# Attention scores over each head's own 64 partitions, one bank per head, queries packed, one score buffer instead of two

## The chip, the core and the metric

The kernel runs on one core of one Trainium2 chip. The metric is the device time of one execution in microseconds (us); lower is better.

## What is computed

Three layers follow one another: windowed attention with block summaries, a mixture of experts with one expert per token, and a Fourier mixing layer with a normalised two-layer network. The change touches only the first. Cut to that part, the reference is:

```python
B, H, S, D = 2, 8, 768, 64          # block 32, window 16
k_sum = k.reshape(B, H, nb, block, D).max(axis=3)
v_sum = v.reshape(B, H, nb, block, D).mean(axis=3)
scores_l = scale * q @ k.T          # kept where |i - j| < 16
scores_s = scale * q @ k_sum.T + log(block)
a = softmax(concat([masked scores_l, scores_s]))
out = a @ concat([v, v_sum])
# then: expert layer on out, then the Fourier layer
```

## The kernel before

The kernel is written engine by engine, with semaphores set and waited for by hand; on each engine, instructions run in the order of the code. The engines are TensorE (PE, whose weight loads stand apart as PEld), VectorE (DVE), ScalarE (ACT), GpSimd (POOL) and SyncE (SP), which issues most transfers.

Attention goes over 8 pairs of heads (`PAIRS`), the two heads of a pair side by side on 128 partitions: head 0 on partitions 0 to 63, head 1 on 64 to 127. Each pair has 6 tiles of 128 queries (`ST`), so there are 48 tiles. The first four pairs run in a loop of two pairs per turn; the last four are written out, and between their tiles stand the gate's logits of the expert layer and the routing that follows from them (`after_probs`, `after_masks`, `after_outputs` on DVE, `beside` on PE).

One tile passes through these steps:

- `scores` (PE, L1697): for each head one matmul of 128 queries against 184 keys (160 in the window, 24 block maxima). The query tile `qT[:, par, hh, ...]` has all 128 partitions, with zeros on the 64 of the other head, so that a contraction over 128 partitions gives one head's scores. An f32 matmul is two passes in the trace, so a tile's scores are four rows of L1697. Both heads of tile t lie side by side in the PSUM bank `S_BANK[t % 2]`.
- `mask_scores` (DVE, L943): adds the mask of each head and takes the row minimum into `masked`; a short read of the accumulator follows each. It signals `masked_ok`.
- exponentials (ACT, L706): two per tile, from `masked` to `probs`, each with a read of its sum.
- `turn_probs` (PE, L1706): three transposes of the probabilities, which DVE copies out (L952, `probs_out`).
- `values` (PE, L1720 to L1722): the product with the values, which DVE normalises (L973).

On PE the step of tile t in a pair is: `turn_probs(t)`, `scores(t + 2)`, for t below 3 a third of the next pair's query and key transposes (`stage`, L1670), work of the gate in the written-out pairs, then `values(t - 1)`. On DVE it is: copy of tile t's transposed probabilities, `mask_scores` of tile t + 2, normalisation of tile t - 1, and after tile 2 the block maxima of the next pair (L932).

`stage` on ACT copies the transposes out of PSUM, scaling the queries: one copy of the first 512 keys (L679), then 256 keys (L683) and 256 queries (L686), then 512 queries (L686). The two L686 copies are each made twice, 64 partitions at a time, since each head has its own zero-padded `qT`. DVE clears `qT` once, at the start (L920).

Of the kernel before, what the change touches and what calls it, by code (L numbers as in the profile page):

```python
# [11 lines left out]
ACT = mybir.ActivationFunctionType  # L12
# [3 lines left out]
B, H, S, D = 2, 8, 768, 64  # L16
BLOCK, WINDOW = 32, 16
DM = H * D
E, FE = 8, 1024
FM = 4 * DM  # L20
P = 128
NB = S // BLOCK
ST = S // P
NT = B * ST
TOK = B * S
PAIRS = B * H // 2
HP = H // 2
SCALE = float(D) ** -0.5


PRE = WINDOW - 1
WK = 160
WB = WK - P
NS = WK + NB
# [12 lines left out]
XW = 516  # L47
# [111 lines left out]
def build(nc, q, k, v, w1, w2, ch1, ch2, consts, four, out):  # L159
    cols = shape_constants()[0]  # L160
    ctx = ExitStack()
    with ctx:
# [28 lines left out]
        mask = const("mask").rearrange("p (v h s) -> p v h s", v=3, h=2)  # L191
# [12 lines left out]
        a = Cut(arena)  # L204
        q_raw = a(ST * P).rearrange("p (t h d) -> p t h d", t=ST, h=2)
        k_raw = a(ST * P).rearrange("p (t h d) -> p t h d", t=ST, h=2)

        qT = a(4 * S).rearrange("p (b h n) -> p b h n", b=2, h=2)
        kT = a(KTW)

        k_win = a(2 * ST * KW).rearrange("p (b t n) -> p b t n", b=2, t=ST)
# [28 lines left out]
        r = Cut(parts)  # L240
# [423 lines left out]
        def _(act):  # L664
# [10 lines left out]
            def stage(i, par, piece):  # L675

                act.wait_ge(qk_ps, 3 * i + piece + 1)
                if piece == 0:
                    act.activation(kT[:, PRE:PRE + 512], Q_BANK[:, :], ACT.Copy).then_inc(qk_sb, 1)  # L679
                    return  # L680
                lo, n, at = (0, 256, 256) if piece == 1 else (256, 512, 0)
                if piece == 1:
                    act.activation(kT[:, PRE + 512:PRE + S], Q_BANK[:, 0:256], ACT.Copy)  # L683
                for hh in range(2):
                    r = slice(D * hh, D * hh + D)
                    last = act.activation(qT[r, par, hh, lo:lo + n], Q_BANK[r, at:at + n], ACT.Copy, scale=-SCALE)  # L686
                last.then_inc(qk_sb, 1)

            def block_mean_rows(i, par):

# [207 lines left out]
        def _(dve):  # L898
# [17 lines left out]


            dve.memset(unspent[:, 0:1], 1.0)
            for tile in (qT, probs, xa[:, :, DM + 2:XW], kT[:, 0:PRE], oh, capped[:, 0:1]):
                dve.memset(tile, 0.0)  # L920
            dve.memset(table_i[:, :], 0)
            link(dve.memset(kT[:, PRE + S:KTW], 0.0))
# [11 lines left out]
            def mask_scores(i, par, t):  # L934

                u = ST * i + t
                slot = 12 * par + 2 * t
                var_ = 0 if t == 0 else 2 if t == ST - 1 else 1
                dve.wait_ge(s_ps, u + 1)
                dve.wait_ge(probs_ok, u + 1)  # L940
                dve.sem_inc(waited, 1)
                for hh in range(2):
                    last = dve.tensor_tensor_reduce(out=masked[:, t % 3, hh, :], in0=S_BANK[t % 2][:, NS * hh:NS * hh + NS], in1=mask[:, var_, hh, :],  # L943
                                                    scale=1.0, scalar=3.0e38, op0=ALU.add, op1=ALU.min, accum_out=neg_max[:, slot + hh:slot + hh + 1])
                last.then_inc(masked_ok, 1)

# [715 lines left out]
        def _(pe):  # L1662
# [25 lines left out]
            def scores(i, par, t):  # L1688
                if t == 0:
                    pe.wait_ge(qk_sb, 3 * i + 3)  # L1690
                    pe.wait_ge(kwin_ok, i + 1)
                    pe.wait_ge(ksum_ok, i + 2)

                pe.wait_ge(masked_ok, ST * i + t + 1)

                for hh, keys in ((0, slice(KS, KW)), (1, slice(0, NS))):
                    last = pe.matmul(S_BANK[t % 2][:, NS * hh:NS * hh + NS], qT[:, par, hh, P * t:P * t + P], k_win[:, par, t, keys],  # L1697
                                     start=True, stop=True)
                last.then_inc(s_ps, 1)

# [85 lines left out]
            def attend(i, par, last_pair):  # L1786
                for t in range(ST):
# [9 lines left out]
                    if t:  # L1797
                        values(i, par, t - 1)
                    if isinstance(i, int) and (i, t) in BEHIND:
                        logits(BEHIND[i, t])  # L1800
                    if isinstance(i, int) and (i, t) in GATE_TURN:
                        turn_gate(GATE_TURN[i, t])
# [259 lines left out]
```

## Time and profile before

| | |
|---|---|
| median of 3 runs | 635.12 us (634.58 to 637.52) |
| time of the profiled execution | 639.09 us |
| its span (first to last instruction) | 637.0 us |
| mean granted TensorE clock | 0.991 |
| PE busy | 604.4 us, 95% |
| PEld busy | 497.5 us, 78% |
| DVE busy | 339.9 us, 53% |
| ACT busy | 248.6 us, 39% |
| POOL busy | 127.1 us, 20% |
| PE's share of the chain that ended last | 78% |

Busy time is the sum of an engine's instructions, overlaps counted once. The span is some 2 us shorter than the time because launch and end lie around it. PE's busy share is an average over three very different layers; what the change is worth has to be read in the attention stage, which ends near 128 us. The chain that ended last goes back from the last instruction, at each step to what released it.

### The profile page before, as it was taken

What the parts mean: (1) busy time and instruction counts of PE and PEld (TensorE: products, weight loads), DVE (VectorE), ACT (ScalarE), POOL (GpSimd) and SP (SyncE); (2) the same over time, 40 slices, a digit from 0 to 9 for tenths busy, and PEclk for the clock granted to TensorE, in tenths of its full rate; (3) what the DMA queues carried; (4) which work ended last, traced back from release to release, by engine and by line L of the source; (5) the groups of instructions that cost most, each with busy time, mean ns of one, the idle gap of its engine ahead of it and who ended that gap; (6) DMA issues with size and microseconds to landing.
All of it is one profiled execution on the core that took longest, in us unless ns stands there. A gap on an engine that the chain in (4) does not pass through costs nothing.

```text
span 637.0 us, 10225 instructions
## 1 busy us (share of the span) xinstructions
PE 604.4 (95%) x3072; PEld 497.5 (78%) x3073; DVE 339.9 (53%) x902; ACT 248.6 (39%) x542; POOL 127.1 (20%) x154
## 2 busy tenths in 40 slices
PE   4899999899989999999799999999999999999997
PEld 3799998788767888888644678888888888888886
DVE  4888679678563564532180665454533344533333
ACT  3588776465132462311011533334333333333331
POOL 5665545403701000000100411200500000200000
PEclk9999999799989999999999999999999999999999
DMA  6967742686536543611232250000010000100001
GB/s 158 167 143 158 157 90 65 242 267 255 204 130 241 179 141 132 241 33 33 99 131 98 101 199 1 1 1 1 26 41 1 2 0 1 66 1 0 2 1 66
DMA packets 59304, 61.68 MB, mean 97 GB/s; under 512 B 42688, under 2 KB 42816, under 8 KB 58240
## 3 DMA queue, kind: packets, MB, share of 16 engines
q1 hardware_dynamic: 54384, 47.21, 25.2%
q0 software_dynamic: 3440, 11.32, 4.7%
q10 hardware_dynamic: 1440, 2.64, 1.4%
q8 instruction: 21, 0.34, 0.3%
q14 instruction: 19, 0.16, 0.1%
HBM read 48.27 MB, written 12.89 MB: 96 GB/s over the span
## 4 chain that ended last, share of the span: by engine, by line
PE 78%; DVE 6%; issue 5%; DMA 4%; ACT 2%; SPq 2%; another core or an unknown queue 1%; POOL 1%; DVEq 0%; ACTq 0%; POOLq 0%
PE bank L2003 21%; PE bank L2016 20%; PE bank L1859 10%; PE bank L1834 9%; PE bank L1697 2%; PE bank L1918 2%; PE bank L1706 1%; ACT arena L706 1%; PE bank L1921 1%; PE bank L1967 1%; DVE parts L1387 1%; PE bank L1846 1%; DMA sorted_x<-zero_row,small 1%; PE bank L1976 1%
## 5 line engine op out<-in xcount | busy, mean ns | idle before, releaser
L2003 PE MATMUL bank<-parts 128*128 128x512 f32 x576 | 139.4, 391 | 1.6 <-DVE parts L1387 1.6
L2016 PE MATMUL bank<-parts 128*128 128x512 f32 x576 | 138.2, 389 | 0.0
L2003 PEld LDWEIGHTS bank<-parts 128*128 128x128 f32 x576 | 107.4, 188 | 24.0 <-DVE parts L1387 1.8
L2016 PEld LDWEIGHTS bank<-parts 128*128 128x128 f32 x576 | 108.1, 188 | 22.5
L1387 DVE TENSOR_TENSOR parts<-arena,parts 128x512 fp32r<-128x512 f32 (+1 forms) x108 | 77.0, 744 | 79.5 <-ACT parts L863 75.8
L1834 PE MATMUL bank<-parts 128*128 128x512 f32 x312 | 77.2, 400 | 2.7 <-issue 1.8
L1859 PE MATMUL bank<-parts 128*128 128x512 f32 x312 | 74.5, 394 | 4.1 <-DVE parts L1387 3.8
L1834 PEld LDWEIGHTS bank<-parts 128*128 128x128 f32 x312 | 58.2, 191 | 16.3 <-issue 4.6
L1859 PEld LDWEIGHTS bank<-parts 128*128 128x128 f32 x312 | 57.6, 188 | 16.6 <-issue 2.5
L863 ACT ACTIVATE parts<-arena 128x512 fp32r<-128x512 f32 x48 | 30.3, 631 | 82.9 <-PE bank L2016 82.9
L1645 DVE SCALAR_TENSOR_TENSOR parts<-bank,parts 128x512 fp32r<-128x512 f32 x48 | 33.2, 691 | 48.2 <-ACT parts L888 48.2
L888 ACT ACTIVATE parts<-bank 128x512 fp32r<-128x512 f32 x48 | 28.7, 598 | 69.3 <-PE bank L2003 67.8
L1387 DVE TENSOR_TENSOR parts<-bank,parts 128x512 fp32r<-128x512 f32 x52 | 34.4, 686 | 27.7 <-ACT parts L853 20.7
L706 ACT ACTIVATE arena<-arena,small 128x184 f32<-128x184 f32 x96 | 42.1, 440 | 16.1 <-DVE small L943 15.3
L1697 PE MATMUL bank<-arena 128*128 128x184 f32 x192 | 41.8, 345 | 1.8 <-ACT arena L686 1.3
L602 POOL DMA_INDIRECT folded_y<-mid,dest_i x13 | 12.6, 973 | 126.7 <-DVE dest_i L1498 126.4
L558 POOL TENSOR_TENSOR mid<-mid 128x1024 f32<-128x1024 f32 (+3 forms) x28 | 33.7, 1204 | 11.9 <-DVE small L1371 8.2
L1697 PEld LDWEIGHTS bank<-arena 128*128 128x128 f32 x192 | 32.6, 207 | 3.0 <-ACT arena L686 1.7
L798 ACT ACTIVATE parts<-bank 128x512 fp32r<-128x512 f32 x26 | 14.1, 594 | 52.5 <-PE bank L1846 40.4
L943 DVE CUSTOM_DVE_ANT_0 arena<-bank,cst 128x184 f32<-128x184 f32 x96 | 29.3, 342 | 9.3 <-PE bank L1697 7.2
L1497 DVE TENSOR_SCALAR mid<-bank,small 128x512 f32<-128x512 f32 x13 | 9.7, 750 | 40.6 <-PE bank L1859 34.5
L858 ACT ACTIVATE parts<-arena 128x512 fp32r<-128x512 f32 x48 | 29.7, 618 | 0.0
(218 smaller groups left out, 764.9 us busy)
## 6 DMA issues: line engine op xcount, KB each, us to landing
mid<-in_moe_w SPq DMA_DIRECT2D x16, 512.0 KB, 6.6
arena<-in_moe_w SPq DMA_DIRECT2D x16, 512.0 KB, 6.5
arena<-in_moe_w_ch SPq DMA_DIRECT2D x2, 2048.0 KB
arena<-in_moe_w_ch SPq DMA_DIRECT2D x4, 1024.0 KB, 9.5
arena<-in_k SPq DMA_DIRECT2D x16, 192.0 KB, 3.2
arena<-in_q SPq DMA_DIRECT2D x16, 192.0 KB, 3.9
mid<-in_v SPq DMA_DIRECT2D x16, 192.0 KB
x_all<-folded_y SPq DMA_DIRECT2D x6, 512.0 KB, 6.4
```

Of the source, the lines that this page charges most:

```text
L558: pool.tensor_tensor(blocks[:, par, 0:n], blocks[:, par, 0:n], blocks[:, par, n:2 * n], ALU.add).then_inc(halved, 1)
L706: last = act.activation(probs[:, t % 3, (2 * NSP - NS) * hh:(2 * NSP - NS) * hh + NS], masked[:, t % 3, hh, :], ACT.Exp, scale=-1.0, bias= ...
L858: act.activation(m1_hi[:, f % 2, :].rearrange("p (c n) -> p c n", c=DC), m1_raw[:, :, P * f:P * f + P], ACT.Copy).then_inc(m1h_ok, 1)
L863: act.activation(m2_hi[:, f % 2, :], m2_raw[:, f, :], ACT.Copy).then_inc(m2h_ok, 1)
L943: last = dve.tensor_tensor_reduce(out=masked[:, t % 3, hh, :], in0=S_BANK[t % 2][:, NS * hh:NS * hh + NS], in1=mask[:, var_, hh, :], scale ...
L1387: return dve.tensor_tensor(out, whole, upper.bitcast(F32), ALU.subtract)
L1645: dve.scalar_tensor_tensor(g_lo[:, f % 2, :], bank[2 + f % 2][:, 0:GN], 0.0, g_hi[:, f % 2, :].bitcast(F32), ALU.max, ALU.subtract).then_i ...
L1697: last = pe.matmul(S_BANK[t % 2][:, NS * hh:NS * hh + NS], qT[:, par, hh, P * t:P * t + P], k_win[:, par, t, keys], start=True, stop=True)
L1834: last = pe.matmul(bank[1 + half][:, :], x[:, r], w[:, c, f], start=(c == 0 and x is xT_hi and w is w1_hi), stop=(c == DC - 1 and w is w1_lo))
L1859: last = pe.matmul(bank[5][:, :], x[:, c, :], w[:, c // 2, f], start=(c == 0 and x is hT_hi and w is w2_hi), stop=(c == FC - 1 and w is w2 ...
L2003: last = pe.matmul(bank[2 + f % 2][:, 0:GN], w[:, f % 2, r], x[:, par, c, :], start=(c == 0 and w is m1_hi and x is cT_hi), stop=(c == DC ...
L2016: last = pe.matmul(bank[4 + t][:, :], x[:, f % 2, r], w[:, f % 2, :], start=(f == 0 and x is g_hi and w is m2_hi), stop=(f == MC - 1 and w ...
```

## The change

Three things change together. The queries of both heads are kept in one packed tile `qT[:, par, n]`, head 0 on the lower 64 partitions and head 1 on the upper 64, and ACT copies both with one instruction; nothing needs zeros any more, so the clearing of `qT` goes. Each score matmul contracts over the 64 partitions of its own head. And each head writes to a bank of its own, `S_BANK[0]` or `S_BANK[1]`, for every tile: two banks still, but one buffer for a tile's scores instead of two. So `scores` of a tile waits until the tile before it is masked, where it waited for the one before that; and the logits that use a score bank in the last pair wait for the last mask.

```diff
-        qT = a(4 * S).rearrange("p (b h n) -> p b h n", b=2, h=2)
+        qT = a(2 * S).rearrange("p (b n) -> p b n", b=2)
...
-                for hh in range(2):
-                    r = slice(D * hh, D * hh + D)
-                    last = act.activation(qT[r, par, hh, lo:lo + n], Q_BANK[r, at:at + n], ACT.Copy, scale=-SCALE)
-                last.then_inc(qk_sb, 1)
+                act.activation(qT[:, par, lo:lo + n], Q_BANK[:, at:at + n], ACT.Copy, scale=-SCALE).then_inc(qk_sb, 1)
...
-            for tile in (qT, probs, xa[:, :, DM + 2:XW], kT[:, 0:PRE], oh, capped[:, 0:1]):
+            for tile in (probs, xa[:, :, DM + 2:XW], kT[:, 0:PRE], oh, capped[:, 0:1]):
...
-                    last = dve.tensor_tensor_reduce(out=masked[:, t % 3, hh, :], in0=S_BANK[t % 2][:, NS * hh:NS * hh + NS], in1=mask[:, var_, hh, :],
+                    last = dve.tensor_tensor_reduce(out=masked[:, t % 3, hh, :], in0=S_BANK[hh][:, 0:NS], in1=mask[:, var_, hh, :],
...
-                pe.wait_ge(masked_ok, ST * i + t + 1)
+                pe.wait_ge(masked_ok, ST * i + t + THREE)
 
                 for hh, keys in ((0, slice(KS, KW)), (1, slice(0, NS))):
-                    last = pe.matmul(S_BANK[t % 2][:, NS * hh:NS * hh + NS], qT[:, par, hh, P * t:P * t + P], k_win[:, par, t, keys],
+                    r = slice(D * hh, D * hh + D)
+                    last = pe.matmul(S_BANK[hh][:, 0:NS], qT[r, par, P * t:P * t + P], k_win[r, par, t, keys],
                                      start=True, stop=True)
                 last.then_inc(s_ps, 1)
...
                     if isinstance(i, int) and (i, t) in BEHIND:
+                        pe.wait_ge(masked_ok, ST * PAIRS + THREE)
                         logits(BEHIND[i, t])
```

Hardly an instruction moves. On TensorE the order in the loop stays; here is the step of tile 3 before (transposes of the probabilities L1706, scores L1697, values L1720 to L1722; bank numbers are those of PSUM):

```order
L1706 MATMUL bank4<-cst,arena 128x128 [waits pT_sb,probs_ok]
L1706 MATMUL bank4<-cst,arena 128x128 x2
L1697 MATMUL bank1<-arena 128x184 [waits masked_ok]
L1697 MATMUL bank1<-arena 128x184
L1720 MATMUL bank5<-arena 128x128 [waits att_out,pT_sb]
L1721 MATMUL bank5<-arena 128x64
L1722 MATMUL bank5<-arena 128x64
```

The same step of the changed kernel, whose lines are renumbered (L1704, L1695, L1718 to L1720):

```order
L1704 MATMUL bank4<-cst,arena 128x128 [waits pT_sb,probs_ok]
L1704 MATMUL bank4<-cst,arena 128x128 x2
L1691 REGISTER_ALU
L1695 MATMUL bank0<-arena 128x184 [waits masked_ok]
L1695 MATMUL bank1<-arena 128x184
L1718 MATMUL bank5<-arena 128x128 [waits att_out,pT_sb]
L1719 MATMUL bank5<-arena 128x64
L1720 MATMUL bank5<-arena 128x64
```

The two score matmuls now go to two banks, and the value that `masked_ok` is waited for is higher by two, which is one tile later: that wait now stands for the mask of the tile just before.

On ScalarE the query copies of a pair (L686 before) stand between the exponentials (L706), before:

```order
L683 ACTIVATE arena<-bank 128x256 [waits qk_ps]
L686 ACTIVATE arena<-bank 64x256 x2
L703 REGISTER_ALU
L706 ACTIVATE arena,small<-arena,small 128x184 [waits pT_ps,masked_ok]
L706 ACTIVATE arena,small<-arena,small 128x184
L677 REGISTER_ALU
L686 ACTIVATE arena<-bank 64x512 [waits qk_ps]
L686 ACTIVATE arena<-bank 64x512
```

and in the changed kernel (L684 and L703):

```order
L683 ACTIVATE arena<-bank 128x256 [waits qk_ps]
L684 ACTIVATE arena<-bank 128x256
L700 REGISTER_ALU
L703 ACTIVATE arena,small<-arena,small 128x184 [waits pT_ps,masked_ok]
L703 ACTIVATE arena,small<-arena,small 128x184
L677 REGISTER_ALU
L684 ACTIVATE arena<-bank 128x512 [waits qk_ps]
```

Two copies of a pair are gone; nothing else moves there.

## Rows read from the trace of the kernel before

**Rows 1.** Busy time by engine in three stretches (calls), granted clock, DMA share, GB/s.
```profile
45.00:70.00 25.00, 24.69 (x200) 24.06 (x199) 20.95 (x96) 20.52 (x69) 16.10 (x26) 1.00 0.73 157
70.00:95.00 25.00, 24.93 (x212) 24.27 (x212) 17.09 (x81) 17.84 (x59) 10.34 (x18) 1.00 0.48 104
95.00:120.00 25.00, 21.42 (x162) 19.89 (x160) 20.84 (x120) 14.49 (x51) 13.97 (x19) 0.95 0.32 99
```

**Rows 2.** The same view, score matmuls alone: PE and PEld busy (passes).
```profile
0.00:20.00 20.00, 4.26 (x12) 3.50 (x12) 1.00 0.79 162
20.00:93.00 73.00, 27.07 (x132) 20.78 (x132) 1.00 0.65 137
93.00:127.00 34.00, 10.46 (x48) 8.28 (x48) 0.90 0.50 157
```

**Rows 3.** Timeline of PE over one pair: start, duration, line, shape, passes.
```profile
44.92 0.79 PE L1697 MATMUL bank<-arena 128*128 128x184 f32 x4
45.54 0.60 PE L1670 MATMUL bank<-cst,arena 128*128 128x128 f32 x4
45.98 0.49 PE L1706 MATMUL bank<-cst,arena 128*128 128x128 f32 x3
46.31 0.79 PE L1697 MATMUL bank<-arena 128*128 128x184 f32 x4
...
50.34 0.79 PE L1697 MATMUL bank<-arena 128*128 128x184 f32 x4
...
51.36 0.39 PE L1722 MATMUL bank<-arena 128*128 128x64 f32 x2
51.91 0.55 PE L1706 MATMUL bank<-cst,arena 128*128 128x128 f32 x3 [0.17 <-ACT arena L706]
52.34 0.89 PE L1697 MATMUL bank<-arena 128*128 128x184 f32 x4
...
56.30 0.79 PE L1697 MATMUL bank<-arena 128*128 128x184 f32 x4
```

**Rows 4.** Timeline of PE in the Fourier layer, rows used*columns of the array ahead of the shape.
```profile
352.55 1.03 PE L1967 MATMUL bank<-arena 128*128 128x258 f32 x4
353.52 0.70 PE L1968 MATMUL bank<-cst,arena 1*128 1x258 f32 x2
354.15 1.14 PE L1976 MATMUL bank<-arena 128*128 128x258 f32 x4
355.12 1.03 PE L1967 MATMUL bank<-arena 128*128 128x258 f32 x4
```

**Rows 5.** Timeline of the weight loads (PEld) at the same place.
```profile
353.52 0.29 PEld L1968 LDWEIGHTS bank<-cst,arena 1*128 1x128 f32 x2 [0.34 <-issue]
354.14 0.73 PEld L1976 LDWEIGHTS bank<-arena 128*128 128x128 f32 x4 [0.34 <-issue]
```

**Rows 6.** Timeline of PE behind six 8-row transposes.
```profile
97.76 0.49 PE L1720 MATMUL bank<-arena 128*128 128x128 f32 x2
98.08 0.33 PE L1721 MATMUL bank<-arena 128*128 128x64 f32 x2
```

**Rows 7.** Groups by line and shape up to 190 us: ACT's copies of `stage`.
```profile
L686 ACT ACTIVATE arena<-bank 64x512 f32<-64x512 f32 x16 | 9.5, 592 | 2.0 <-PE bank L1670 1.8
L686 ACT ACTIVATE arena<-bank 64x256 f32<-64x256 f32 x16 | 6.0, 372 | 0.1
L679 ACT ACTIVATE arena<-bank 128x512 f32<-128x512 f32 x8 | 4.8, 598 | 10.4 <-PE bank L1670 10.4
```

**Rows 8.** Timeline of DVE, last reads of the masks of tiles 2 and 5.
```profile
46.55 0.08 DVE L943 DVE_READ_ACCUMULATOR2_ANT small<- 128x1 f32 x1
...
52.53 0.08 DVE L943 DVE_READ_ACCUMULATOR2_ANT small<- 128x1 f32 x1
```

**Rows 9.** Timeline of the start.
```profile
1.46 2.62 DVE L920 MEMSET arena<- 128x3072 f32 x1 [0.61 <-issue]
...
6.28 0.60 ACT L679 ACTIVATE arena<-bank 128x512 f32<-128x512 f32 x1 [0.39 <-PE bank L1670]
...
20.36 0.90 PE L1670 MATMUL bank<-cst,arena 128*128 128x128 f32 x3 [2.88 <-DMA arena<-in_k]
```

**Rows 10.** The chain that ended last, in order of time, behind the attention.
```profile
121.55 7.45 DMA sorted_x<-zero_row,small
...
134.17 5.79 DMA arena<-in_moe_w
```

## The prediction

> **What bounds the kernel now.** I read the busy time by stretch first, because the average over three layers says nothing of one stage. From 45 to 95 us PE is busy 24.7 and 24.9 of every 25 us, while DVE has 17 to 21 and ACT 18 to 21 [rows 1]: the first two thirds of the attention are PE's alone. From 95 to 120 us PE falls to 21.4 and DVE has 20.8: there the two take turns, because routing work stands between the masks. Counting score passes by the same stretches, four to a tile, 3 tiles are computed before 20 us, 33 from 20 to 93, and 12 after [rows 2]. The wait that ends the start is a transfer: PE stands at 20.36 us for the second pair's keys [rows 9], so whatever happens before that is worth nothing. Behind the attention the chain goes through the clearing of rows (7.45 us) and the first expert weights (5.79 us) [rows 10]; both are triggered by the routing that is threaded through the last pairs, and the weights also wait for the last scores, since they overwrite the attention's buffers. So I carry a shift of the attention to the end one for one.
>
> Then the timeline of one pair in the loop, from scores at 44.92 to the same place at 56.30: 11.38 us [rows 3]. Starts, not durations, give the pace. Scores 44.92 to 45.54: 0.62 us for four passes of 184 columns, 0.155 each, with no gap, so the weight loads are hidden. `stage` takes 0.44, the transposes 0.33. Once per pair PE waits: the values' last two passes start at 51.36 and pace out at about 51.58, the next transposes start at 51.91, 0.33 us late, released by an exponential; they and the scores behind them take 0.43 and (from the duration, 0.89 for 0.79) 0.72 instead of 0.33 and 0.62. That is some 0.5 us of waiting and restarting per pair.
>
> **The change part by part.**
>
> *Scores over 64 rows.* No row of this kernel uses 64 rows. The nearest are matmuls over 1 row between matmuls over 128 [rows 4]. Undisturbed, 258 columns pace at 0.217 us a pass: (1.03 − 0.38)/3, where 0.38 is the last pass's duration. From 352.55 to 355.12 there are ten passes, 2.17 us, but 2.57 us go by. The 0.40 us of excess splits into about 0.10 behind L1967 (0.97 for four), 0.20 in L1968 (0.63 for two) and 0.10 in L1976 (0.97 for four). The loads show why: the first load of L1968 and of L1976 starts together with the matmul, 0.34 us after the load before it [rows 5], where elsewhere it is done ahead. The array empties (about 0.1), then loads uncovered (about 0.1), once going in and once coming out. The 8-row transposes show the second half too: L1720 behind them takes 0.32 instead of the usual 0.22 [rows 6]. Each tile's scores now stand between 128-row work on both sides, so each pays this: +0.40 us.
>
> The Trainium skill, "TensorEngine Tiling (Array Packing)", Key Properties, says the same: changing the tiling mode, not just the tile, drains TensorE. By that rule 64 rows would pay as 1 row does; by a reading in which only a very short contraction pays, the term would be nothing. The rows decide only for 1 and 8 rows.
>
> Against that stands overlap. The two heads now use different halves of the array. The passes come in the order head 0, head 0, head 1, head 1. If a pass can run beside one of the other half but starts in order, only the second and third overlap: at most one pass, 0.155 us. None is the other bound. The loads (0.11 us each, by the pace of the transposes) must also come one after another: head 1's first load, the third in the row, ends at 0.33 us, while the second pass runs from about 0.26 to 0.42. Some 0.1 is left to overlap; I take 0.10. Net per tile: +0.30, between +0.245 and +0.40.
>
> *Waits inside a pair.* The 0.5 us that PE waits now for the exponential is absorbed: PE comes later by more than that, and ACT comes earlier, since the second 64-partition query copies go. A copy costs the same over 64 as over 128 partitions (592 and 598 ns), so ACT saves 0.59 + 0.37 = 0.96 us per pair [rows 7]. Beyond the absorbed wait this is worth nothing, ACT having 4 us of idle in 25.
>
> Now the single buffer. `scores(3)` must wait for the mask of tile 2, which ends at 46.63 against scores at 46.31; the first scores of the next pair wait for the mask of tile 5, which ends at 52.61 against 52.34 [rows 3, 8]. With 0.05 for the signal these are 0.37 and 0.32 us late in today's schedule. Elsewhere in a pair `values` and longer steps stand between, and the mask is done. What is queued behind the waiting scores is everything of PE: the transposes, the values, and through them DVE's normalisation. In the new schedule PE reaches `scores(3)` up to 0.3 us later than now while the mask moves less, so that wait shrinks; at the next pair's first scores PE is held up by 0.3 more per tile but no longer by the exponential, so that wait stays. I take 0.5 per pair for both, between 0 and 0.75. It cancels the absorbed 0.5.
>
> So +0.30 × 6 = +1.8 us per pair, 0.30 per tile. For 33 tiles: +9.9. For the 12 tiles behind 93 us PE has room, but a slower score also delays the mask that DVE waits for; I take half, 0.15: +1.8, between 0 and 0.40 each.
>
> *The rest.* The clearing of 3072 columns, 2.62 us of DVE, is gone; the first key copy of ACT waits for PE's transposes until 6.28 anyway, and PE stands for the transfer at 20.36 [rows 9]: nothing. Were that transfer 2 us earlier, it would still be nothing. The added waits before two logits in the last pair stand where the last masks are long done. The DVE masks keep size and number.
>
> Sum: 9.9 + 1.8 = 11.7 us. On the profiled execution, 639.09 becomes 650.8. That execution is 4.0 us above the median of 635.12; on the median the same sum gives **646.8**, forecast 647.
>
> **The rivals.**
>
> *Slower, as above (0.75).* Its own range: low, one full pass of overlap (+0.245), no new waits while 0.5 a pair is absorbed (−0.08 a tile), nothing in the last 12: 33 × 0.16 = 5.3, so 640.4. High, no overlap (+0.40), waits of 0.75 a pair less 0.5 absorbed (+0.04), and the last 12 in full: 33 × 0.44 + 12 × 0.40 = 19.3, so 654.4.
>
> *Faster: the heads run side by side (0.12).* If 64-row tiles neither drain nor expose loads, and both passes of one head run beside those of the other, scores take 0.31 instead of 0.62. For it: the layout, halves of the array and separate banks, is what such overlap needs. Against it: the order of passes and [rows 4]. PE would gain 0.31 a tile, but would then meet the mask sooner: about 0.17 a tile goes into the single buffer's waits. 45 × 0.14 = 6.3, so 629. It decides when entering and leaving costs less than about 0.15 us a tile together. The Trainium skill, "TensorE: Matmul & The Clock Gate", Part 3, speaks for it: matmuls of different row groups are said to start about 4 ns apart. No row here shows it.
>
> *No change (0.13).* The switch is free or nearly so, and one pass overlaps: −0.155 a tile, given back by the new waits (0.75 a pair, 0.125 a tile). 45 × −0.03 = −1.4, so 634. The same result comes if both heads overlap fully and the switch costs 0.15. For it: the switch is seen only at 1 and 8 rows.
>
> **How the numbers follow.** About 0.5%, 3.2 us, is what a measurement of this kernel can tell from none. The range must leave out no more than 2 in 10: it leaves out the faster rival and a little above the high bound, and takes in no change from 637 and up: 637 to 655. Almost all of the likeliest case is over 638.3: slower 0.75, same 0.13, faster 0.12.
>
> **What would show it.** In the changed profile: scores marked 64*128; from the first score pass to the next group's start 0.7 to 0.8 us instead of 0.62; the first load of scores and that of the group behind starting with their matmuls, with idle before them; 12.8 to 13.6 us a pair instead of 11.38; PE waiting for the mask before `scores(3)` and the next pair's first; ACT's L684 at 16 calls instead of 32, no time won by it. Wrong would be: score starts of the two heads a few ns apart, or loads still hidden at the change of rows (then the faster rival); or a pair near 11.4 us with new waits for the mask (no change); or a delay of the attention that the weight transfers swallow.

## The result, and the profile after

| | before | after |
|---|---|---|
| median of 20 runs | 635.75 us (632.72 to 640.04) | 638.37 us (636.14 to 640.72) |
| ratio, with its 95% interval | | 1.0041 (1.0026 to 1.0056) |
| time and span of the profiled execution | 639.09 and 637.0 us | 638.82 and 636.8 us |
| PE, DVE, ACT busy | 604.4, 339.9, 248.6 us | 603.1, 338.2, 240.5 us |

The change costs 2.6 us, 0.4%: slower, but within the 0.5% that I had called no change. I had forecast 11.7 us more. Medians and ratios in this document leave out the executions that ran in a slower state of the chip, three of the ten of `maxima_earlier_copies_as_before` and one of the kernel before beside them.

The busy time by stretch, in the changed kernel; the columns are those of [rows 1].

```profile
45.00:70.00 25.00, 23.81 (x193) 18.97 (x192) 20.07 (x91) 17.88 (x66) 15.51 (x24) 1.00 0.73 155
70.00:95.00 25.00, 25.00 (x211) 21.34 (x209) 16.37 (x79) 15.62 (x52) 10.10 (x18) 1.00 0.39 87
95.00:120.00 25.00, 22.27 (x181) 17.63 (x181) 23.26 (x126) 14.37 (x52) 14.97 (x21) 1.00 0.41 116
```

In the loop's stretch PE is busy for 23.8 of 25 us where it was 24.7: PE now waits, and not for a transfer. Timeline of PE around the pair of [rows 3]. The rows begin one tile earlier than those did: 44.08 is the place that is 42.67 in the kernel before (scores of this pair's tile 1), and the next scores, at 46.41, are those that stood at 44.92.

```profile
44.08 0.58 PE L1695 MATMUL bank<-arena 64*128 64x184 f32 x4
...
47.41 0.49 PE L1704 MATMUL bank<-cst,arena 128*128 128x128 f32 x3
48.08 0.58 PE L1695 MATMUL bank<-arena 64*128 64x184 f32 x4 [0.18 <-DVE small L940]
48.59 0.66 PE L1667 MATMUL bank<-cst,arena 128*128 128x128 f32 x4
49.09 0.39 PE L1718 MATMUL bank<-arena 128*128 128x128 f32 x2
...
51.75 0.50 PE L1704 MATMUL bank<-cst,arena 128*128 128x128 f32 x3
52.18 0.58 PE L1695 MATMUL bank<-arena 64*128 64x184 f32 x4
52.69 0.49 PE L1718 MATMUL bank<-arena 128*128 128x128 f32 x2
53.02 0.33 PE L1719 MATMUL bank<-arena 128*128 128x64 f32 x2
...
53.41 0.50 PE L1704 MATMUL bank<-cst,arena 128*128 128x128 f32 x3
54.42 0.58 PE L1695 MATMUL bank<-arena 64*128 64x184 f32 x4 [0.51 <-DVE small L940]
...
56.08 0.58 PE L1695 MATMUL bank<-arena 64*128 64x184 f32 x4
```

The shape 64*128 says that half of the array's rows are used. Three readings of starts:

- Scores last 0.51 us to the next group (52.18 to 52.69), where they lasted 0.62. They got shorter.
- The transposes ahead of them last 0.43 (51.75 to 52.18), where 0.33 was usual: +0.10. The values behind them take 0.33 for their first two passes (52.69 to 53.02), where 0.22 was usual: +0.10. With `stage` behind them it is 0.50 (48.59 to 49.09) for 0.44: some +0.05.
- Scores come late twice, for the mask (L940). The scores of tile 3: 47.41 + 0.43 is 47.84, and they start at 48.08, 0.24 late. The first scores of the next pair: 53.41 + 0.43 is 53.84, and they start at 54.42, 0.58 late. No wait for an exponential is left.

The weight loads at the same place show the rest of it:

```profile
51.64 0.37 PEld L1704 LDWEIGHTS bank<-cst,arena 128*128 128x128 f32 x3
52.18 0.30 PEld L1695 LDWEIGHTS bank<-arena 64*128 64x128 f32 x4 [0.17 <-issue]
52.69 0.30 PEld L1718 LDWEIGHTS bank<-arena 128*128 128x128 f32 x2 [0.21 <-issue]
```

The loads of scores and of the group behind both start together with their matmuls, as at the one-row matmuls of [rows 5]: the array empties first, and then the first load is uncovered, going in and coming out.

The rows above merge the four passes of a tile's scores. Taken one by one, the trace has their starts at 52.181, 52.187, 52.441 and 52.447 us, and those of their loads at 52.179, 52.186, 52.287 and 52.294. The passes come in twos, 6 ns apart, and so do the loads. The trace doesn't say which head a pass is of; I take one of each two for each head. A start of the two heads a few ns apart is what the prediction had named as the sign that it was wrong.

The pair from 44.08 to 56.08 takes 12.00 us for 11.38. The other pairs of the loop that show in full take 11.82 and 11.83; the wait at the scores of tile 3 is only 0.07 there, the other one as long as here. In the written-out pairs, taken from scores of tile 2 to scores of tile 2, the steps are 18.22, 14.26 and 14.16 for 18.05, 13.76 and 14.14.

A wait stands at the start too, in the first pair, just behind the transfer of the second pair's keys. The kernel before:

```profile
20.36 1.12 PE L1670 MATMUL bank<-cst,arena 128*128 128x128 f32 x4 [2.88 <-DMA arena<-in_k]
21.91 1.44 PE L1697 MATMUL bank<-arena 128*128 128x184 f32 x4
```

and the changed kernel:

```profile
19.87 1.11 PE L1667 MATMUL bank<-cst,arena 128*128 128x128 f32 x4 [3.80 <-DMA arena<-in_k]
22.56 0.98 PE L1695 MATMUL bank<-arena 64*128 64x184 f32 x4 [0.93 <-DVE small L940]
```

From the first transposes behind the transfer to the scores of tile 3 it is 2.69 us for 1.55. DVE is as late in both kernels, since it computes block means until then, but with two buffers PE did not have to wait for it. So 1.1 us of the loss arise before the loop is under way.

Where all that leads, in rows of the timelines, first of the kernel before:

```profile
91.98 0.79 PE L1697 MATMUL bank<-arena 128*128 128x184 f32 x4
107.10 0.94 DVE L932 TENSOR_REDUCE arena<-arena 128x24 f32<-128x768 f32 x1
...
116.23 0.29 DVE L973 TENSOR_TENSOR x_all<-bank,small 128x128 f32<-128x128 f32 x1 [2.58 <-remote]
```

and of the changed kernel:

```profile
95.00 0.58 PE L1695 MATMUL bank<-arena 64*128 64x184 f32 x4
110.24 0.94 DVE L929 TENSOR_REDUCE arena<-arena 128x24 f32<-128x768 f32 x1
```

The same scores come 3.0 us later, and the last block maxima 3.1 us later. Read at a tile's scores, the shift is 1.05 us early in the second pair (33.54 and 34.59), 2.6 three pairs on (67.67 and 70.24) and 3.3 at 113.62 and 116.88. The medians differ by 2.6 us, so most of that shift reaches the end; as medians and profile are of different executions, no row shows it being carried. The two profiled spans, 637.0 and 636.8, don't show the loss, because the execution profiled of the kernel before lost 2.58 us at 116.23 to a wait whose cause the trace only calls remote. PE stood still behind it for 2.05 us, and its granted clock from 117 to 124 us was 0.53, for 1.00 in the changed kernel. The other profile has no such wait. So the medians are compared for the sum, and not these two spans.

### The profile page after: what moved, and what is told of

It reads as the page before. It is cut to its first block, busy times and chain, and to the rows that moved or that the text cites. A ratio compares the mean times of both kernels' runs of the same rounds, so it can differ in the third digit from the quotient of the medians.

```text
span 636.8 us, 10206 instructions
## 1 busy us (share of the span) xinstructions
PE 603.1 (95%) x3072; PEld 478.9 (75%) x3073; DVE 338.2 (53%) x901; ACT 240.5 (38%) x526; POOL 127.4 (20%) x154
## 4 chain that ended last, share of the span: by engine, by line
PE 84%; DVE 5%; DMA 4%; issue 4%; ACT 1%; POOL 1%; DVEq 0%; SPq 0%; ACTq 0%; POOLq 0%
PE bank L2002 21%; PE bank L2015 20%; PE bank L1858 11%; PE bank L1833 10%; PE bank L1695 2%; PE bank L1917 2%; PE bank L1667 2%; DMA x_all<-sorted_x 2%; PE bank L1920 1%; PE bank L1718 1%; PE bank L1845 1%; PE bank L1966 1%; DMA sorted_x<-zero_row,small 1%; PE bank L1736 1%; PE bank L1704 1%
## 5 line engine op out<-in xcount | busy, mean ns | idle before, releaser
L703 ACT ACTIVATE arena<-arena,small 128x184 f32<-128x184 f32 x96 | 42.0, 440 | 19.2 <-DVE small L940 18.6
L1695 PE MATMUL bank<-arena 64*128 64x184 f32 x192 | 29.6, 386 | 7.1 <-DVE small L940 6.2
L940 DVE CUSTOM_DVE_ANT_0 arena<-bank,cst 128x184 f32<-128x184 f32 x96 | 29.5, 344 | 7.3 <-PE bank L1695 3.9
L949 DVE COPY arena<-bank 128x384 f32<-128x384 f32 x48 | 26.5, 552 | 3.2 <-PE bank L1704 2.5
```

The lines of the kernel that those rows point to most:

```text
L703: last = act.activation(probs[:, t % 3, (2 * NSP - NS) * hh:(2 * NSP - NS) * hh + NS], masked[:, t % 3, hh, :], ACT.Exp, scale=-1.0, bias= ...
L1695: last = pe.matmul(S_BANK[hh][:, 0:NS], qT[r, par, P * t:P * t + P], k_win[r, par, t, keys], start=True, stop=True)
```

## The experiments

Each median stands beside runs of the kernel before on the same chip, and the ratio is to those. The pair times are from scores of tile 1 to scores of tile 1 of the next pair (44.08 to 56.08 above), the three of the loop that show in full; before, they are 11.38 us each.

| kernel | median us | ratio to before | us a pair |
|---|---|---|---|
| after | 638.37 | 1.0041 (1.0026 to 1.0056) | 11.82, 12.00, 11.83 |
| single_buffer_only | 642.43 | 1.0104 (1.0084 to 1.0125) | 12.31, 12.38, 12.30 |
| each_head_twice | 652.05 | 1.0232 (1.0199 to 1.0266) | 13.78, 13.80, 13.77 |
| copies_and_clearing_as_before | 640.38 | 1.0060 (1.0040 to 1.0080) | 11.83, 12.00, 11.82 |
| four_banks_in_loop | 639.34 | 1.0056 (1.0038 to 1.0074) | 11.69, 11.94, 11.70 |
| scores_behind_values | 648.03 | 1.0190 (1.0168 to 1.0213) | 12.21 each |
| block_maxima_earlier | 635.75 | 0.9986 (0.9967 to 1.0005) | 11.25, 11.42, 11.25 |
| maxima_and_mask_earlier | 635.36 | 0.9977 (0.9957 to 0.9996) | 11.24, 11.25, 11.25 |
| before_with_dve_moves | 638.78 | 1.0030 (1.0014 to 1.0046) | 11.99 each |
| before_with_maxima_earlier | 643.79 | 1.0030 (0.9992 to 1.0068) | 12.06, 11.99, 11.99 |
| maxima_earlier_copies_as_before | 645.36 | 1.0074 (1.0044 to 1.0104) | 12.05, 12.23, 12.04 |

For the last two the kernel before beside them took 642.26 and 640.70 us, so that only their ratios and pair times compare with the others.

### How the heads overlap

**single_buffer_only** is the kernel before with one buffer and a bank for each head, still over 128 rows: the part that was to cost waits, alone.

```diff
-                pe.wait_ge(masked_ok, ST * i + t + 1)
+                pe.wait_ge(masked_ok, ST * i + t + THREE)
-                    last = pe.matmul(S_BANK[t % 2][:, NS * hh:NS * hh + NS], qT[:, par, hh, P * t:P * t + P], k_win[:, par, t, keys],
+                    last = pe.matmul(S_BANK[hh][:, 0:NS], qT[:, par, hh, P * t:P * t + P], k_win[:, par, t, keys],
```

> The kernel before with one part of the change: each head has a score bank of its own for every tile and so one buffer, but scores still contract over 128 partitions with zero-padded queries, and ACT's split copies stay. Theory: in the changed kernel the waits for the mask are what costs, about 0.7 us a pair, since PE stands at the scores of tile 3 and at the next pair's first. Then this one is slower than before by 3 to 6 us (639 to 642), and its scores take 0.62 us a tile as before, with two waits for a mask per pair of 0.3 us each. Rival: the wait is absorbed by the wait for the exponential, and the switch of rows is the whole cost: 635 to 637.

It measured 12.3 us a pair and a ratio of 1.0104: slower than the whole change. Scores were late for the mask twice a pair, and the transposes at 56.06, 0.31 us behind the pace, still stand for the exponential (the gap is too short for a bracket):

```profile
50.38 0.89 PE L1697 MATMUL bank<-arena 128*128 128x184 f32 x4 [0.22 <-DVE small L943]
...
55.53 0.39 PE L1722 MATMUL bank<-arena 128*128 128x64 f32 x2
56.06 0.55 PE L1706 MATMUL bank<-cst,arena 128*128 128x128 f32 x3
56.84 0.89 PE L1697 MATMUL bank<-arena 128*128 128x184 f32 x4 [0.23 <-DVE small L943]
```

So one buffer costs 0.9 to 1.0 us a pair by itself, and the rest of the change wins 0.4 to 0.5 of it back, although by the rows above it gives PE 0.3 to 0.4 us a pair more to do: what shrinks is the waiting. (The query copies have no part in that: copies_and_clearing_as_before, below.) In my forecast the halved rows were the loss and the buffer nothing on balance; the larger loss is the buffer's. No run has the halved rows with the two score buffers of the kernel before and all else as it was.

**each_head_twice** computes each head's scores twice over, in the order head 0, head 0, head 1, head 1 (eight passes; the second result replaces the first).

```diff
-                    last = pe.matmul(S_BANK[hh][:, 0:NS], qT[r, par, P * t:P * t + P], k_win[r, par, t, keys],
-                                     start=True, stop=True)
+                    for _ in range(2):
+                        last = pe.matmul(S_BANK[hh][:, 0:NS], qT[r, par, P * t:P * t + P], k_win[r, par, t, keys],
+                                         start=True, stop=True)
```

> The changed kernel with each head's score matmul issued twice in a row into the same bank (the second repeats the first), so the order is head 0, head 0, head 1, head 1 by instruction, eight passes a tile. It asks how the passes of the two halves of the array overlap. Theory: each half works through its own passes regardless of the order in the code, so eight passes take four pass times, 0.62 us, and the scores take 0.51 + 0.31 = 0.82 us from their start to the next group's; whole kernel about 12 us over the changed one, 648 to 652. Rival: only passes that are neighbours overlap (head 0's second with head 1's first), so that of four instructions the outer two run alone: 0.31 + 0.31 + 0.31 + 0.2 = 1.13 us a tile; 660 and over.

Timeline of PE:

```profile
56.31 0.90 PE L1696 MATMUL bank<-arena 64*128 64x184 f32 x8
57.14 0.66 PE L1667 MATMUL bank<-cst,arena 128*128 128x128 f32 x4
```

Eight passes take 0.83 us from start to start, four took 0.51: four more passes for 0.32, two passes' time. Had the four passes of head 1 started only behind the last of head 0, at most one would have been hidden: 7 × 0.155 + 0.2 is 1.29; my rival's 1.13 is excluded too. One by one the passes again start in twos, 13 ns apart: 56.310 and 56.323, 56.570 and 56.583, 56.726 and 56.739, 56.882 and 56.895. The halves each work through their own passes, whatever stands between them in the code.

**both_heads_lower_half** takes head 1's operands from the lower 64 partitions too. It computes scores from head 0's data twice and none of head 1's; so the attention's output differs, the routing with it, and only its attention stage can be read. It was measured twice.

```diff
-                    r = slice(D * hh, D * hh + D)
+                    r = slice(0, D)
```

> The changed kernel with the second head's score matmul reading partitions 0 to 63 as well (so the second head's scores are computed from the first head's data). Same number of passes, same 64-row shape, same banks and waits, but both heads use the same half of the array and can't run side by side. Theory: the changed kernel's 0.51 us a tile holds two pass times (0.31) and 0.2 of drain and load; without overlap four pass times: 0.82 us. 45 tiles by 0.31 is 14 us, less what the waits for the mask take back: 647 to 653. Rival (the prediction's bound, at most one pass overlaps): 0.66 us a tile, 643 to 646. Rival (64 rows are simply cheap, no overlap in it): 638, no change.

> The kernel with both heads' scores on partitions 0 to 63 once more (second head's scores computed from the first head's data), for a trace with TensorE at its full pace in the attention. Only the attention is read, since the routing depends on the data. Theory: 0.82 us from the start of a tile's scores to the next group's, 0.31 more than in the changed kernel, and about 13 us a pair. Rival (at most one pass had overlapped): 0.66 us.

The first time its six executions took 649.5 to 703.08 us, so that the forecast of 647 to 653 says nothing, and in the profiled one PE was at half pace through the loop, until about 100 us: 24.1 us a pair. The second time (one execution, 659.17 us) that lasted until about 56 us, timelines of PE and of the weight loads:

```profile
47.60 1.59 PE L1695 MATMUL bank<-arena 64*128 64x184 f32 x4
49.12 1.11 PE L1667 MATMUL bank<-cst,arena 128*128 128x128 f32 x4
...
56.36 0.90 PE L1695 MATMUL bank<-arena 64*128 64x184 f32 x4
57.19 0.49 PE L1718 MATMUL bank<-arena 128*128 128x128 f32 x2
...
56.36 0.61 PEld L1695 LDWEIGHTS bank<-arena 64*128 64x128 f32 x4 [0.33 <-issue]
```

From 56.36 on the pace is the usual one, and there four passes on one half last 0.83 us, against 0.51 on two halves. That is 0.32 or two passes, with the same switch, the same number of loads and the same banks: the overlap is that of the halves, and it is whole. The four loads span 0.61 us on one half and 0.30 on two, so they run side by side as well. The pair takes 13.7 us there where I expected about 13; up to 1.1 us of it is the lengthened DVE operation described under before_with_maxima_earlier.

### Where the new wait comes from

**four_banks_in_loop** gives the pairs of the loop two score buffers again (four banks), taking a bank from the transposed probabilities, which keep one.

```diff
+        def score_bank(i, t, hh):
+            return (bank[2], bank[4])[hh] if looped(i, t) and t % 2 else S_BANK[hh]
...
-                pe.wait_ge(masked_ok, ST * i + t + THREE)
+                pe.wait_ge(masked_ok, ST * i + t + (1 if looped(i, t) else THREE))
```

> The changed kernel with two buffers of scores for the four pairs of the loop: odd tiles use PSUM banks 2 and 4, and the transposed probabilities use bank 3 alone there. The last four pairs are as in the changed kernel. Theory: the waits for the mask at scores go in the loop, some 0.7 us a pair, in 3.5 pairs: 11.2 to 11.4 us a pair instead of 12.0, 635.5 to 637. Rival: the single buffer costs nothing, or DVE's masks are late anyway and the wait only moves to the transposes: 638, no change.

```profile
52.61 0.52 PE L1714 MATMUL bank<-cst,arena 128*128 128x128 f32 x3 [0.33 <-DVE arena L959]
53.06 0.58 PE L1705 MATMUL bank<-arena 64*128 64x184 f32 x4
```

No wait for a mask is left in the loop. The transposes wait for DVE's copy of the ones before (L959) in its place, and the pair is shorter by 0.1 us only. DVE was late, and whichever bank it has to free next shows it. By itself this run can't tell whether banks are scarce, since one of the two that the scores got was taken from the transposes; block_maxima_earlier, below, shows that one buffer will do once DVE is earlier.

**scores_behind_values** puts `scores(t + 2)` at the end of PE's step, behind `values(t - 1)`, so that the mask has longer.

```diff
-                    if t + 2 < ST:
-                        scores(i, par, t + 2)
...
+                    if t + 2 < ST:
+                        scores(i, par, t + 2)
```

> The changed kernel with PE's order in a tile's step changed: scores of tile t + 2 stand behind the values of tile t - 1 instead of ahead of them, still single-buffered. Theory: PE does 0.6 us of other work before it needs the mask, so the waits for the mask go, while the exponential of tile t + 2 still has more than a tile's time: 633 to 636. Rival: the mask, the exponential and with them the transposes come 0.6 us later, and the wait only moves from scores to transposes, or grows: 638 to 642.

```profile
53.85 0.58 PE L1695 MATMUL bank<-arena 64*128 64x184 f32 x4
54.74 0.55 PE L1704 MATMUL bank<-cst,arena 128*128 128x128 f32 x3 [0.31 <-ACT arena L703]
```

Later scores make a later mask and a later exponential, and the transposes wait instead, here and once more in each pair (0.21 us at 56.94). The pair takes 12.21 us and the ratio is 1.0190. The loop explains 1 to 2 of some 9.5 us by which this kernel is slower than the changed one; the rest lies behind the loop, where among others three waits of 0.45 us for ACT (L736) come up at 81.54, 85.16 and 88.79, and was not taken apart.

**block_maxima_earlier** changes only DVE: the block maxima of the next pair (0.95 us, once a pair) go ahead of the normalisation of tile 1 instead of behind it.

```diff
+                    if t == 2 and not last_pair:
+                        block_max(i + 1, 1 - par)
                     if t:
                         normalise(i, par, t - 1, out_at(t - 1))
                     if isinstance(i, int):
                         after_outputs(i, t)
-                    if t == 2 and not last_pair:
-                        block_max(i + 1, 1 - par)
```

> The changed kernel with one thing moved on DVE: the block maxima of the next pair stand ahead of the normalisation of tile 1 instead of behind it, where DVE idles 0.5 us for the values. Theory: they and all behind them come 0.5 us earlier, so the mask of tile 5 is done when PE reaches the next pair's first scores, and that wait (0.58 us a pair) goes: 11.4 to 11.5 us a pair instead of 12.0, 634 to 636. Rival: the wait moves on to the transposes of tile 5, which need the exponential: 637 to 638.5.

The reason is in DVE's timeline of the changed kernel:

```profile
52.06 0.29 DVE L970 TENSOR_TENSOR x_all<-bank,small 128x128 f32 x1 [0.49 <-PE bank L1720]
52.28 0.95 DVE L929 TENSOR_REDUCE arena<-arena 128x24 f32<-128x768 f32 x1
...
53.21 0.55 DVE L949 COPY arena<-bank 128x384 f32<-128x384 f32 x1
...
53.76 0.32 DVE L940 CUSTOM_DVE_ANT_0 arena<-bank,cst 128x184 f32<-128x184 f32 x1
```

DVE stands 0.49 us for the values, then does the maxima, and only then the copy and the mask for which PE's scores at 54.42 wait. With the maxima in the idle time (49.84 there, ahead of L970 at 50.71), the time is that of the kernel before (0.9986, 0.9967 to 1.0005), and PE's rows at the same places are

```profile
51.77 0.50 PE L1704 MATMUL bank<-cst,arena 128*128 128x128 f32 x3
52.20 0.58 PE L1695 MATMUL bank<-arena 64*128 64x184 f32 x4
52.72 0.49 PE L1718 MATMUL bank<-arena 128*128 128x128 f32 x2
```

with no wait for the next pair's first scores. The pair takes 11.25 us, or 11.42 where the scores of tile 3 wait (0.18 idle at 46.44). That is about what the terms give without a new wait: 11.38 − 0.5 (the old wait) + 0.4 (rows) = 11.28.

**maxima_and_mask_earlier** adds a second move on DVE in the loop: the mask of tile 2 ahead of the copy of tile 0.

> As the kernel before it in this call, and in the loop's pairs the mask of tile 2 stands ahead of the copy of tile 0's transposed probabilities instead of behind it. Theory: that mask starts when its scores are done, 0.2 us earlier, and PE's wait at the scores of tile 3 (0.1 to 0.24 us) goes as well: 0.1 to 0.2 us a pair less than the kernel with the maxima alone in four pairs, a difference too small to be told in the time (under 1 us) but seen in the pair's period. Rival: the copies come later and PE waits for them at the values or transposes: equal or longer period.

It makes all pairs 11.25 and the ratio 0.9977 (0.9957 to 0.9996). That is ahead of the kernel before by 0.2%, barely clear of its interval, and not to be told from the maxima alone.

### Whether the kernel before could have the same

**before_with_dve_moves** is the kernel before with both moves, and **before_with_maxima_earlier** with that of the maxima alone.

> The control: the kernel before, with the same two moves on DVE (block maxima ahead of the normalisation of tile 1, mask of tile 2 ahead of the copy of tile 0). Theory: the kernel before doesn't wait for masks, so the moves are worth nothing there (within 1 us of before, 11.3 to 11.4 us a pair), and what they won in the changed kernel was the price of the single buffer. Rival: the moves shorten DVE's work order as such and win 2 to 3 us here too, so that the changed layout is no better than before with them.

> The kernel before with one of the two moves on VectorE alone: the block maxima of the next pair ahead of the normalisation. It has two score buffers, so its masks are not waited for by TensorE, and its one wait of 0.5 us a pair is for an exponential. If the loss of the kernel before with both moves (11.99 us a pair) came from the mask of tile 2 going ahead of the copy of tile 0, then this kernel keeps 11.38 us a pair and 636 us, within 0.3%. If the block maxima are what harms it (the normalisation later by a microsecond, hence the values and the exponentials), the pair stays near 12.0 us and the time near 639. If they help it as they helped the changed kernel, the pair falls to 11.2 and the time to 634, and then the changed kernel with the same move has nothing that the kernel before could not have.

Both take 11.99 us a pair for 11.38: the move that helps the changed kernel lengthens the pair of the one before, and the maxima alone do it. The time of the first is 0.3% up; that of the second has the same ratio, but an interval that reaches 1. DVE's timeline of the second, and below it ACT's:

```profile
55.01 1.18 DVE L960 TENSOR_SCALAR small<-small 128x4 f32<-128x4 f32 x1
56.11 0.55 DVE L952 COPY arena<-bank 128x384 f32<-128x384 f32 x1
```

```profile
53.83 0.19 ACT L706 ACTIVATION_READ_ACCUMULATOR arena<-arena,small 128x1 f32 x1
...
55.12 0.45 ACT L706 ACTIVATE arena<-arena,small 128x184 f32<-128x184 f32 x1
...
55.91 0.19 ACT L706 ACTIVATION_READ_ACCUMULATOR arena<-arena,small 128x1 f32 x1
```

L960 is an operation of 0.16 us on the exponentials' sums of tiles 4 and 5. Here it holds DVE for 1.18, the copy behind it is late, and PE waits for that copy (0.48 us at 56.71). The expectations call this a wait for the sums, and the rows say otherwise: the read that ends tile 5's exponentials is over at 54.02, and DVE passed the semaphore that stands for it at 54.84, ahead of L960. What runs beside L960 is the exponential of the next pair's tile 0 (55.12 to 56.10), whose sums it doesn't read. In the loops of five kernels the operation took 1.14 to 1.27 us, 19 times, two kernels with packed copies among them (each_head_twice and both_heads_lower_half_again). Each time it had started between 0.18 us ahead of that exponential and 0.04 us behind its start, and it ended 0.1 to 0.3 us behind its last read. In the changed kernel it starts 0.30 us ahead (56.17 and 56.47) and takes 0.16. So the loss hangs on where two engines' operations meet in time. What holds the operation is not shown.

**copies_and_clearing_as_before** is the changed kernel with each query copy made twice, 64 partitions at a time, and with the clearing; **maxima_earlier_copies_as_before** has the earlier maxima too.

```diff
-                act.activation(qT[:, par, lo:lo + n], Q_BANK[:, at:at + n], ACT.Copy, scale=-SCALE).then_inc(qk_sb, 1)
+                for hh in range(2):
+                    r = slice(D * hh, D * hh + D)
+                    last = act.activation(qT[r, par, lo:lo + n], Q_BANK[r, at:at + n], ACT.Copy, scale=-SCALE)
+                last.then_inc(qk_sb, 1)
```

> The changed kernel with ACT's query copies split into two of 64 partitions again and with 3072 columns cleared at the start again; nothing of PE's or the banks is touched. Theory: neither was worth anything, since PE waits for DVE's masks and not for ACT, and the start ends with a transfer: 638 to 639.5, no change beyond 1 us. Rival: the packed copies shorten the path to the exponentials of tile 4 and with it pay for part of the rest: 641 to 643, and waits of PE for ACT of 0.3 us a pair come back.

> The changed kernel with the block maxima ahead of the normalisation (which alone gave 11.25 to 11.42 us a pair) and with the query copies made twice, 64 partitions at a time, and the queries cleared, as before. In the kernel before, the same move of the block maxima made a pair 11.99 us: there the query copies of 1.19 us stand between the exponentials, and the check of the exponentials' sums waited 1.1 us with the copy of the last transposes behind it. If the longer query copies are what turns the move into a loss, this kernel shows about 11.9 us a pair, that wait of VectorE again, and a time near 639. If the copies are hidden here too (they made no difference to the pair without the move: 11.83 and 12.00 against 11.82 and 12.00), the pair stays at 11.25 to 11.4 and the time near 636, and the loss of the kernel before with the move comes from its slower scores over 128 rows.

Without the move the doubled copies change no pair (11.83, 12.00, 11.82); the ratio is 0.2% (1.2 us) above that of the changed kernel, with intervals that overlap, so it stays open whether the clearing at the start is worth anything. With the move they cost 0.8 us a pair (12.05 for 11.25). ACT's timeline of that kernel, and below it DVE's:

```profile
52.57 1.20 ACT L687 ACTIVATE arena<-bank 64x512 f32<-64x512 f32 x2
...
57.10 0.45 ACT L707 ACTIVATE arena<-arena,small 128x184 f32<-128x184 f32 x1
...
57.89 0.19 ACT L707 ACTIVATION_READ_ACCUMULATOR arena<-arena,small 128x1 f32 x1
```

```profile
57.05 1.14 DVE L961 TENSOR_SCALAR small<-small 128x4 f32<-128x4 f32 x1
```

The long operation of 1.1 us on DVE is back, beside the next pair's first exponential as in the kernel before. So the packed copies are what lets the earlier maxima pay here: doubled, the copies cost a pair nothing while DVE is late, and 0.8 us once it is not. The 0.8 is not ACT's 0.96 us handed on, but the price of that meeting; whether another shift of ACT's work would avoid it as well was not tried.

## Why the prediction was wrong

**The step that failed** is the overlap: "If a pass can run beside one of the other half but starts in order, only the second and third overlap: at most one pass, 0.155 us." I took 0.10, because the loads "must also come one after another". Neither holds. The runs show 0.31, both passes of one head beside both of the other: 0.51 us for scores on two halves and 0.83 on one, and eight passes in 0.83 where the order rule gave 1.29. The four loads span 0.30 us on two halves and 0.61 on one. The order of passes in the code was taken for the order in which they start. With 0.31 in place of 0.10, and nothing else touched, my own sum is 0.09 a tile: 33 × 0.09 + 12 × 0.045 = 3.5 us for the 2.6 measured. That it comes so near is in part luck, as smaller errors below go both ways.

**The range**, 637 to 655, holds 638.37 only by its low end, which I had added for the case of no change; the bounds of my own case, 640.4 to 654.4, leave it out. That is no success of the forecast.

**The switch of rows**, 0.40 us a tile from [rows 4, 5], was right in its parts: 0.10 on the transposes, 0.10 uncovered at the start of scores (0.51 is two passes, 0.31, and 0.2 around them, of which 0.1 the emptying), 0.10 on the values behind. Only with `stage` behind is it about 0.05 less. The one-row matmuls were a good stand-in for 64 rows. The Trainium skill, "TensorEngine Tiling (Array Packing)", Key Properties, which says that a change of mode drains, agrees with these rows (the 0.10 ahead of the scores).

**The old wait absorbed**, 0.5 us a pair: right; no wait for an exponential is left.

**The new waits**, 0.5 a pair between 0 and 0.75, at `scores(3)` and at the next pair's first: the places were right, the size low. In the pair shown they are 0.24 and 0.58, together 0.82, and in the other pairs 0.07 and 0.57. The sum 11.38 + 0.4 − 0.5 + 0.8 gives 12.1 for 12.00, and with 0.6 it gives 11.9 for 11.8: 0.1 too much both times. That the first would shrink, from 0.37, was right. The second did not stay at 0.32 but grew, and for it I had named the mask alone as late. What DVE does once a pair, the block maxima, stands between the values and that mask, and I had not put it there; moved away, it took the wait with it.

**ACT's 0.96 us worth nothing**: right for the pairs of this kernel, by the copies as before. The reason I gave, that ACT has idle time, does not hold in general: the packed copies are worth 0.8 us a pair in the kernel whose DVE is not late.

**The last 12 tiles**, 1.8 us, cost 0.1 to 0.3: 3.0 us at 95.00, 3.1 at 110.24, 3.3 at 116.88; behind that the lost 2.58 us of the other profile hide the rest. **The start** at nothing was wrong: PE stood for the transfer as I said, but right behind it the single buffer cost 1.1 us. **The shift carried one for one** fits, 2.6 us by the medians for 3.1 to 3.3 in the profiles, without a row that shows it.

**The rivals.** The faster one had the overlap right and named its own threshold, 0.15 us a tile for going in and out; the switch costs 0.35 to 0.40, so that it could not come true. The Trainium skill, "TensorE: Matmul & The Clock Gate", Part 3, lets matmuls of different row groups start about 4 ns apart. The trace, with 6 and 13 ns, agrees, and I should have weighed this higher against the order of passes. The case that happened, whole overlap and the whole price of the switch, was in none of my cases: I had tied the high switch to the small overlap, though nothing ties them.

## What to carry to other kernels

Price the overlap and the price of entering it as two unknowns, and work out all four corners; here the corner left out was the one that came. In this kernel two halves of the array saved half the passes' time, 0.31 us of four passes of 184 columns, and cost 0.35 to 0.40 us each time, since full-height work stands on both sides; the passes saved would have to be more than that. When an engine waits on a bank, look at what the engine that frees it does just before, above all at what it does once in many steps: moving 0.95 us of it took 0.6 us off a pair, a second score buffer that took a bank from the transposes 0.1.

## What the runs showed of the hardware

- The two halves of TensorE's rows take their passes independently of the order in the code: head 0 four passes, head 1 four passes, in 0.83 us, in which one half by itself does four.
- With both heads on the lower half, PE ran at half pace until 56 us in one execution and 100 us in another (scores 1.52 us for 0.83), while the granted clock in the profile stood at 1.00, which is the 2.4 GHz level. The windows of both_heads_lower_half_again:

```profile
30.00:45.00 15.00, 15.00 (x59) 12.45 (x58) 6.87 (x29) 5.41 (x19) 5.63 (x7) 1.00 0.37 80
```

  PE is busy throughout, with few instructions. Every kernel here starts at that pace, with 1.00 recorded, and all others leave it between 24 and 28 us: in the kernel before, the scores at 21.91 take 1.23 us to the next group and those at 25.56 take 0.63. Elsewhere the record does show such a pace, as 0.53 behind the lost 2.58 us of the kernel before, where a tile's scores (119.83) again take 1.23. So the rows look like the lower of the two clock levels in spite of the record. Why this kernel alone stays there for so long no run tells.
- An operation of 0.16 us on four columns (L960 on DVE) took 1.14 to 1.27 us when it started beside the start of an exponential on ACT. Its inputs were ready, the trace counts it as busy all the time, and no bracket names a releaser.
